# GpSimd block sums over two k tiles instead of one, in the two down projections

## The reference

```python
kv = einsum('bhsd,bhse->bhde', softmax(k, over s), v)
x  = einsum('bhsd,bhde->bhse', softmax(q, over d), kv)      # [4608, 512]
h  = silu(x @ w_gate) * (x @ w_val)                         # d_ff 1536
y  = h @ w_out                                              # [4608, 512]
g  = elu(y @ w_in)                                          # d_ff 2048
out = g @ w_out2                                            # [4608, 512]
```

## Time and profile before

| | |
|---|---|
| runs | 1893.96 us median of three (1893.53 to 1895.43) |
| the profiled execution | 1893.53 us; its span in the trace 1891.7 us |
| busy | TensorE 1735.7 us (92%), VectorE 1283.6 us (68%), GpSimd 788.3 us (42%), ScalarE 765.5 us (40%) |
| instructions on GpSimd | 513, of which 280 are the block sums of B and D |

### The profile page before, as it was taken

The page is one execution under the profiler, slowest core; times in us unless marked ns, Lnnn a source line. Parts: engine busy times, 40 slices in busy tenths (PEclk is TensorE's granted clock), DMA queues, the critical chain, the costliest instruction groups (busy, mean ns, idle before and its releaser), DMA issues.

```text
span 1891.7 us, 22530 instructions
## 1 busy us (share of the span) xinstructions
PE 1735.7 (92%) x8024; PEld 1465.7 (77%) x8024; DVE 1283.6 (68%) x1694; ACT 765.5 (40%) x1240; POOL 788.3 (42%) x513
## 2 busy tenths in 40 slices
PE   7998989898989899999999879999999889999898
PEld 6776777776777788878888768889889767778787
DVE  6747474746464612298888748797886787878876
ACT  4333242424243311245555435454454434445443
POOL 5623323231313331167566924152240365563745
PEclk9999999999999999999999989999999899999999
DMA  7745565657575556643435382442417843625241
GB/s 190 206 151 165 180 195 151 196 162 205 147 211 166 157 190 211 233 167 134 159 127 191 126 314 94 154 152 88 156 78 289 344 114 97 184 62 146 89 116 30
DMA packets 314832, 308.73 MB, mean 163 GB/s; under 512 B 142432, under 2 KB 277088, under 8 KB 311904
## 3 DMA queue, kind: packets, MB, share of 16 engines
q1 hardware_dynamic: 314720, 307.29, 50.2%
HBM read 172.49 MB, written 134.74 MB: 162 GB/s over the span
## 4 chain that ended last, share of the span: by engine, by line
PE 42%; DVE 21%; issue 3%; DMA 2%; ACT 1%; SPq 0%; ACTq 0%; DVEq 0%
PE psum L931 14%; PE psum L933 14%; PE psum L932 14%; DVE g_lo L1457 9%; DVE h_lo L1457 7%; DVE g_rows L1534 2%; DMA hidden_T<-g_rows 1%; DVE g_rows L1532 1%; DMA layer_out_T<-y_low 1%; DVE g_parts L1520 1%; ACT g_hi L1201 1%; DVE y_top L1470 0%; PE psum L954 0%; DVE kv_lo L1401 0%; ACT h_hi L1201 0%
## 5 line engine op out<-in xcount | busy, mean ns | idle before, releaser
L931 PE MATMUL psum<-x_hi,weights 128*128 128x512 f32 x864 | 346.1, 401 | 4.4 <-DVE x_lo L1426 3.9
L933 PE MATMUL psum<-x_lo,weights 128*128 128x512 f32 x864 | 339.7, 393 | 0.0
L932 PE MATMUL psum<-x_hi,weights 128*128 128x512 f32 x864 | 339.2, 393 | 0.0
L1457 DVE TENSOR_TENSOR g_lo<-g_raw,g_hi 128x448 fp32r<-128x448 f32 (+1 forms) x280 | 282.7, 1051 | 58.8 <-ACT g_hi L1201 58.5
L1445 DVE TENSOR_TENSOR hid<-psum,act_out 128x512 f32<-128x512 f32 x108 | 74.6, 691 | 288.4 <-PE psum L933 216.4
L931 PE MATMUL psum<-g_hi,g_w 128*128 128x448 f32 (+1 forms) x560 | 221.4, 395 | 35.9 <-DVE g_lo L1457 35.5
L1457 DVE TENSOR_TENSOR h_lo<-h_raw,h_hi 128x448 fp32r<-128x448 f32 (+1 forms) x210 | 229.5, 1145 | 23.1 <-ACT h_hi L1201 22.9
L931 PE MATMUL psum<-y_hi,w_in_f 128*128 128x448 f32 (+1 forms) x560 | 210.0, 375 | 24.9 <-ACT g_parts L1260 24.9
L1201 ACT ACTIVATE g_hi<-g_raw 128x448 fp32r<-128x448 f32 (+1 forms) x280 | 164.6, 591 | 149.1 <-PE psum L933 138.6
L932 PE MATMUL psum<-g_hi,g_w 128*128 128x448 f32 (+1 forms) x560 | 212.9, 380 | 0.0
L933 PE MATMUL psum<-g_lo,g_w 128*128 128x448 f32 (+1 forms) x560 | 212.5, 379 | 0.0
(11 more groups left out here) (113 smaller groups left out, 3124.8 us busy)
## 6 DMA issues: line engine op xcount, KB each, us to landing
hidden_T<-hid SPq DMA_DIRECT2D x108, 256.0 KB, 3.4
forms_w_out<-fact_forms SPq DMA_DIRECT2D x28, 896.0 KB, 6.3
hidden_T<-g_rows SPq DMA_DIRECT2D x48, 448.0 KB, 2.7
g_raw<-hidden_T SPq DMA_DIRECT2D x12, 1792.0 KB, 8.0
h_raw<-hidden_T SPq DMA_DIRECT2D x12, 1344.0 KB, 8.7
hidden_T<-g_rows SPq DMA_DIRECT2D x32, 480.0 KB, 2.9
g_raw<-hidden_T SPq DMA_DIRECT2D x8, 1920.0 KB, 8.3
forms_w_in<-fact_forms SPq DMA_DIRECT2D x32, 448.0 KB, 5.4
```

The lines of the kernel that those rows point to most:

```text
L931: pe.matmul(acc, w_hi, xh, start=start, stop=False, skip_group_check=goes_on)
L932: pe.matmul(acc, w_lo, xh, start=False, stop=False, skip_group_check=goes_on)
L933: return pe.matmul(acc, w_hi, xl, start=False, stop=stop, skip_group_check=goes_on)
L1457: dve.tensor_tensor(of.lo[t % of.ring][:, 0:n], of.block(of.slot_of(p, i), n)[:, kt, :], of.hi[t % of.ring][:, 0:n].bitcast(F32), ALU.subt ...
```

## The change

The class `Down` now takes two k tiles per chunk. Each of the four series has 3 instructions in stage B instead of 6, and 4 in stage D instead of 8; each covers `[128 x 896]` or `[128 x 960]`. All waits that are counted in chunks follow: ScalarE waits for the chunk that holds its tile, and line 868 waits until two k tiles of form 3 are split. Nothing else is changed.

```diff
@@ class Down: __init__
                 self.kt = kt
-                self.chunk = 1
-                self.chunks = kt
+                self.chunk = 2
+                self.chunks = kt // 2
                 self.ring = ring
```

## The result

The changed kernel takes 1959.79 us (median of four, 1955.87 to 1962.51), the kernel before 1894.7 us on the same chip (1893.53 to 1903.09): a ratio of 1.0332, 95% interval 1.0295 to 1.0369. The change makes it slower by some 63 us (the ratio of all runs; the two medians are 65 us apart). I had forecast slower, 1937 us, with 1952 as the upper end of the range: the sign was right and the size was not. The profiled executions, 1893.53 and 1956.46 us, differ by 62.9, and their spans by 63.0.

What follows compares the result with a forecast made beforehand. TensorE was taken to bound the kernel, with VectorE setting the pace in a stretch of each pair. Terms 30 (stage D) + 6.5 (clock) + 7 (stage B) = 43.5 us on 1893.53 gave 1937.0 us, range 1920 to 1952.

Steps and rivals of the forecast that it cites:

- What bounds the kernel: Whole kernel: TensorE, busy for 92% of the span, sets the pace, but in each pair there is a stretch where VectorE does.
- The longer turn: VectorE's subtractions beside GpSimd's two-tile sums: a step of 2.45 us instead of 1.50 at 448 tokens, 2.64 at 480.
- Stage D, forms 4 and 5, with the clock: Five pairs: form 4 later, form 5 returning part, 30 us; low clock in form 4's second pass, 6.5 us.
- Stage B: Form 5's second pass starts 1.4 us later in each pair; 7 us over five pairs.
- the next pair's series: Stage D, line 862's sums: few VectorE tiles beside them, and five tiles end where they ended before; cost nothing.
- Loads move with TensorE: Loads into the next pair's blocks wait for adds and turns, so they shift with TensorE; no size given.
- The bound for that case: Line 862's series starting onto a full VectorE queue: two more steps, 2 us a pair.
- The faster: Rival: VectorE isn't held for the whole long sum and steps 1.42 us instead of 1.50; 1880 us, chance 0.04.
- the equal: Rival: VectorE gets two subtractions per long sum, mean step 1.53 us; 1895 us, chance 0.04.
- the slower-by-less one: Rival: in half of form 4's steps VectorE waits for things other than the lock; 1915 us, chance 0.12.
- The clock's rival: Rival: form 4's second pass in stage D runs at half clock throughout; 1952 us, chance 0.15.

## Why the prediction was wrong

- *What bounds the kernel* was right: TensorE, and VectorE in a stretch of each pair. The loss is in those stretches.
- *The longer turn.* Right in mechanism and size. I took 2.45 us a step; four sums at line 873 start to line 877's start in 9.42 us, and the eight subtractions took 19.60. The experiment with single instructions under the same waits takes the loss away. By the Trainium skill ("SBUF — State Buffer", section "Summary: rules for kernel authors") the second of two such instructions to issue blocks until the first one finishes; the trace agrees in the main, at three lengths (steps of 1.00, 1.50 and 2.45 us beside 224, 448 and 896 elements). The two durations alone (0.65, 1.14 or 2.12 us for the sum, 0.61 for the subtraction) add up to 1.26, 1.75 and 2.73, so some 0.25 us of each pair does overlap.
- *Stage D, forms 4 and 5, with the clock.* I had 30 + 6.5 = 36.5 us; the passes of these forms lost 35.9, of which form 4's second passes, where I put the clock, have 4.6.
- *Stage B.* I had 7 us, it lost 4.4. Form 5's second pass starts 15.1 us after form 4's first in the fourth pair (1021.16 and 1006.02), where it was 14.1: 1.0 us a pair, not 1.4. The path was as I had it: form 5's first pass starts 2.4 us later (I had 2.6), and the second pass no longer waits.
- *The step that failed* is the one on the next pair's series: "I cost it at nothing; if its start fell onto a full VectorE queue, two more steps would be 2 us a pair." It did fall there, in four of five pairs, and the first passes of form 0 lost 25.8 us, 6 us in each of these pairs. A pair of 448 tokens takes 91.4 us from form 4 to form 4 where I had 87. The reason stands further on in the prediction: "Loads move with TensorE". They do not all do so. The load behind line 877 moved with GpSimd, which I had myself called through before form 5, and twelve stores and the load for line 862 stood behind it. I costed the faster engine's effect on VectorE and not what it triggers. Held back by one wait, the changed kernel takes 1936.95 us, ratio 1.0207; the forecast's 1937 was a ratio of 1.023. That the two times agree to a tenth is luck: there D lost 31.5 us and B 4.4, for 36.5 and 7 in my sum.
- *The bound for that case* was mis-sized too. I counted two steps, 2 us a pair. In the fourth pair all four long sums met the split, and its eight tiles take 11.98 instead of 4.9 us, of which TensorE's pass feels 4.3 us, and 2.4 us of low clock come on top.
- *The rivals.* The faster, the equal and the slower-by-less one had nothing in them: beside long sums the subtractions stepped 2.45 us on average over form 4, none of them at 1.5. The clock's rival is part of the surprise, but in another pass: form 4's second passes lost 4.6 us in all, form 0's first ones about 8. That the 1952 of that rival lies nearest to the measurement is luck.

That form 0's low clock comes from thin work is not shown. It stayed away in the fourth pair when the last tile was as late but the tiles came evenly, 1.5 us apart; but it also stayed away in the third pair of the kernel with two-tile sums in D alone, where the tiles came as in the changed kernel (that pass took 8.8 us, in the changed kernel 10.5).

## What to carry to other kernels

Before grouping small instructions on an engine, look at what a neighbouring engine's instruction does beside one that is already long in the same trace: the price stood in the kernel's own rows. When an engine gets faster, follow every count that it raises, into the DMA queues too, and ask what starts earlier and on whose queue it falls. And a neighbour's busy share that holds turns waited for is no measure of its load: giving the "busy" engine more work made the kernel 4% faster.

## What the runs showed of the hardware

An engine with 140 more instructions to execute was busy for 71 us less, because a subtraction's wait for its turn is counted in its duration. The turns cut both ways. With sums of half a tile the subtractions step 1.0 us, and GpSimd, at 2.0 us a k tile beside VectorE, becomes the late one. The lower clock level came in form 0's first pass after 4 us in which TensorE was busy for 1.64, and it stayed for 6.8 us, though TensorE was busy for 5.06 of 6 us of them, by matmuls at that level.
